# Moving half copies, sums, gates and one low half in a one-core attention and expert kernel

## What is computed

```
mask = q_bucket == k_bucket                 # 6 sign bits of q @ proj and of k @ proj
scores = where(mask, q @ k.T / 8, -1e9)
attn = exp(scores - max) / (sum + 1e-9);  x = attn @ v      # (1536, 512)
x = (sigmoid(x @ w_gate) * (x @ w_val)) @ w_out             # hidden width 1536
h = x @ w_in
g = where(h >= 1, h, where(h <= -1, 0, (h + 1)**2 / 4))     # hidden width 2048
out = g @ w_out2
```

## Time and profile before

| | |
|---|---|
| median of 3 runs | 792.86 us (792.75 to 793.1) |
| the profiled execution, its span | 792.82 us, 790.7 us |
| PE busy | 775.2 us, 98% |
| VectorE, ScalarE, GpSimd busy | 551.3 (70%), 461.5 (58%), 538.5 (68%) |
| chain that ended last | PE 79%, VectorE 6%, ScalarE 6%, issue 4%, GpSimd 4% |
| PE clock in 40 slices | 9 tenths or more in each |

### The profile page before, as it was taken

The page is one execution under the profiler, slowest core; times in us unless marked ns, Lnnn a source line. Parts: engine busy times, 40 slices in busy tenths (PEclk is TensorE's granted clock), DMA queues, the critical chain, the costliest instruction groups (busy, mean ns, idle before and its releaser), DMA issues.

```text
span 790.7 us, 12182 instructions
## 1 busy us (share of the span) xinstructions
PE 775.2 (98%) x4403; PEld 717.3 (91%) x4403; DVE 551.3 (70%) x862; ACT 461.5 (58%) x731; POOL 538.5 (68%) x533
## 2 busy tenths in 40 slices
PE   7999999999999999999999999999999999999998
PEld 6899999998989999999899999988899988899996
DVE  5888888888888666555765655577677776766554
ACT  4888988988997443344453334356455465634443
POOL 4567667778889988877596977747756755465420
PEclk9999999999999999999999999999999999999999
DMA  6895586385100222022021211121121011201002
GB/s 146 181 197 131 136 168 141 79 163 131 55 1 1 80 81 81 29 78 80 27 81 54 80 54 63 44 80 54 32 77 54 29 51 40 95 27 54 1 1 80
DMA packets 61930, 60.08 MB, mean 76 GB/s; under 512 B 28384, under 2 KB 51632, under 8 KB 61872
## 3 DMA queue, kind: packets, MB, share of 16 engines
q1 hardware_dynamic: 61712, 59.32, 28.5%
q10 hardware_dynamic: 160, 0.00, 0.0%
HBM read 37.75 MB, written 3.15 MB: 52 GB/s over the span
## 4 chain that ended last, share of the span: by engine, by line
PE 79%; DVE 6%; ACT 6%; issue 4%; POOL 4%; DMA 0%; SPq 0%; DVEq 0%; POOLq 0%; ACTq 0%
PE ps L748 12%; PE ps L749 11%; PE ps L750 11%; PE ps L777 8%; PE ps L789 5%; PE ps L790 5%; PE ps L788 5%; PE ps L778 4%; PE ps L714 4%; ACT ph L906 2%; PE ps L731 2%; PE ps L732 2%; PE ps L702 2%; DVE probs L1207 2%; PE ps L705 2%
## 5 line engine op out<-in xcount | busy, mean ns | idle before, releaser
L748 PE MATMUL ps<-xop,wset 128*128 128x384 f32 x560 | 191.0, 341 | 4.1 <-DVE u L1282 2.1
L749 PE MATMUL ps<-xop,wset 128*128 128x384 f32 x560 | 189.3, 338 | 0.0
L750 PE MATMUL ps<-xop,wset 128*128 128x384 f32 x560 | 188.8, 337 | 0.0
L1282 DVE TENSOR_TENSOR u<-ps,u 128x384 f32<-128x384 f32 x144 | 79.6, 553 | 109.0 <-PE ps L750 108.3
L516 POOL TENSOR_TENSOR wset<-stage,wset 128x512 fp32r<-128x512 f32 x39 | 56.5, 1448 | 112.7 <-ACT wset L953 112.7
L748 PEld LDWEIGHTS ps<-xop,wset 128*128 128x128 f32 x560 | 105.2, 188 | 18.0 <-issue 3.8
L1218 DVE TENSOR_TENSOR pl<-ps,ph 128x768 fp32r<-128x768 f32 x96 | 91.5, 954 | 26.5 <-ACT ph L906 25.4
L749 PEld LDWEIGHTS ps<-xop,wset 128*128 128x128 f32 x560 | 105.4, 188 | 3.5
L491 POOL TENSOR_SCALAR probs<-probs,small 128x768 f32<-128x768 f32 x96 | 88.4, 927 | 24.9 <-DVE small L1212 22.1
L750 PEld LDWEIGHTS ps<-xop,wset 128*128 128x128 f32 x560 | 105.2, 188 | 0.0
L522 POOL TENSOR_TENSOR wset<-wsum,wset 128x1024 fp32r<-128x1024 f32 x39 | 95.3, 2443 | 0.0
(11 more groups left out here) (134 smaller groups left out, 1710.4 us busy)
## 6 DMA issues: line engine op xcount, KB each, us to landing
stage<-in_moe_w_in_dram SPq DMA_DIRECT2D x16, 512.0 KB, 3.6
stage<-in_moe_w_out_dram SPq DMA_DIRECT2D x14, 512.0 KB, 3.6
stage<-in_moe_w_gate_dram SPq DMA_DIRECT2D x12, 512.0 KB, 4.3
stage<-in_moe_w_val_dram SPq DMA_DIRECT2D x12, 512.0 KB, 3.5
ops<-qh SPq DMA_DIRECT2D x15, 384.0 KB, 5.3
ops<-kh SPq DMA_DIRECT2D x28, 192.0 KB, 5.1
qn<-in_q_dram SPq DMA_DIRECT2D x16, 192.0 KB, 4.5
kn<-in_k_dram SPq DMA_DIRECT2D x16, 192.0 KB, 5.0
```

Of the source, the lines that this page charges most:

```text
L748: pe.matmul(dst, high[:, c, :], high_x(r)[:, c, :], start=(c == 0), stop=False)
L749: pe.matmul(dst, high[:, c, :], low_x(r)[:, c, :], start=False, stop=False)
L750: last = pe.matmul(dst, low[:, c, :], high_x(r)[:, c, :], start=False, stop=(c == 1))
L1282: dve.tensor_tensor(dst, bank(n, r), other, ALU.add).then_inc(e_dve, 1)
```

## The change

Seven edits. In attention ScalarE's `copy_half` for u = 5, 8, 11 moves from ahead of the step's cast and exponential to behind them; at u = 2 it stays ahead. In pair 5 GpSimd's three pieces of the first sums come at u = 1, 4, 7 instead of 4, 7, 10. GpSimd's `low_wo` of set 25 (f = 4) comes in set 26. In sets 24 and 32 ScalarE takes relu and square together ahead of the next set's first product, which goes back into that set, and VectorE adds the hinge ahead of the next set's bank 1. Value sets next to a first set gate their second half in two parts of 384 columns, the first of them ahead of `empty(n, 5)`. The sums ahead of the second and third first set (12 and 24) move from sets 3, 4, 5 behind a first set to 4, 6, 8.

```diff
-                if i == NP - 3 and u in (4, 7, 10):
-                    first_sum(0 if u == 4 else 2, (u - 7) // 3)
+                if i == NP - 3 and u in (1, 4, 7):
+                    first_sum(0 if u == 4 else 2, u // 7)
...
-                if WO2 + 1 < n <= WO2 + T2 + 1 and n % 2:
+                if WO2 + 1 < n <= WO2 + T2 + 1 and (n % 2 and n != N1 + 1 or n == N1 + 2):
                     f = (n - WO2 - 2) // 2
                     low_wo(T1 // 2 + f, f, (narrow2(2 * f), narrow2(2 * f + 1)))
...
             def hinge_set(n):
-                if n - 1 not in FIRSTS:
-                    first_product(n)
+                first_product(n)
                 if n in FIRSTS:
                     round_w(n + 1)
                     empty_y(g - 1)
-                    hinge_relu(t)
-                    first_product(n + 1)
-                    hinge_square(t)
+                    hinge_part(t)
                     return
...
-                if g % HT == 2 and g >= 11:
+                if u == 2 and g >= 11:
                     copy_half((g - 11) // HT)
...
                 exponential(g)
                 if g % HT == 2 and g >= 11:
+                    if u != 2:
+                        copy_half((g - 11) // HT)
                     copy_other((g - 11) // HT)
...
+            def gate_half(n):
+                two = hidden(pair_of(n), 1)
+                dve.wait_ge(sig_done, 2 * pair_of(n) + 1)
+                dve.wait_ge(*emptied(n, 4))
+                dve.tensor_tensor(two[:, G:S], two[:, G:S], tmp[:, G:S], ALU.mult)
+            def gate_other(n):
+                two = hidden(pair_of(n), 1)
+                dve.wait_ge(*emptied(n, 5))
+                dve.tensor_tensor(two[:, 0:G], two[:, 0:G], tmp[:, 0:G], ALU.mult).then_inc(gated, 1)
...
-                if g < 3 and n - FIRSTS[g] in (3, 4, 5):
-                    sum_x(g + 1, n - FIRSTS[g] - 3)
+                at = (4, 6, 8) if g < 2 else (3, 4, 5) if g == 2 else ()
+                if n - FIRSTS[g] in at:
+                    sum_x(g + 1, at.index(n - FIRSTS[g]))
...
                 empty(n, 4)
-                sum_ahead(n)
-                empty(n, 5)
                 if n - 1 in FIRSTS or n + 1 in FIRSTS:
-                    gate_second(n)
+                    gate_half(n)
+                    empty(n, 5)
+                    gate_other(n)
                     empty(n, 6)
                 else:
+                    empty(n, 5)
                     empty(n, 6)
                     gate_second(n)
...
                 empty(n, 6)
+                add_hinge(t)
                 if n in FIRSTS:
                     empty(n + 1, 1)
-                add_hinge(t)
                 clamp(t + 1)
```

More of the change, by code:

```diff
@@ L992, in sigmoids, with hinge_part @@
                     act.activation(hidden(pp, second), hidden(pp, second), ACT.Sigmoid).then_inc(sig_done, 1)
-            def hinge_relu(t):
+            def hinge_part(t):
                 act.wait_ge(clamped, t - TILES1 + 1)
                 act.activation(tile(t), tile(t), ACT.Relu, bias=minus_one).then_inc(hinge_parts, 1)
-            def hinge_square(t):
                 act.activation(tmp[:, :], tmp[:, :], ACT.Square, bias=half, scale=0.5).then_inc(hinge_parts, 1)
-            def hinge_part(t):
-                hinge_relu(t)
-                hinge_square(t)
             def empty_y(g):
```

## The result

The changed kernel takes 803.15 us (median of four runs, 802.77 to 804.83) against 792.81 (792.38 to 793.1) for the kernel before on the same chip: a ratio of 1.0137, interval 1.0122 to 1.0152. That is 1.2 us above the forecast of 802.0 and inside the range. The profiled execution took 803.02, with a span of 801.2 where the one before had 790.7. First the page: span, busy time by engine, and the chain of work that ended last.

What follows compares the result with a forecast made beforehand. TensorE, busy 98% of the span at full clock, was taken as the bound. Terms +2.8 - 0.95 + 2.3 - 0.7 - 0.9 + 6.6 = +9.15 on 792.86 gave 802.0 us, range 796 to 805.5.

Steps and rivals of the forecast that it cites:

- copies: Attention: ScalarE's moved half copies make the key turn late in six pairs, 0.46 us each; +2.8 us.
- first sums: Attention, pair 5: the GpSimd piece at u = 10 moves to u = 1, where the queue has room; -0.95 us.
- gate halves, sets 1 and 13: Each half gate waits for a whole GpSimd instruction, delaying PE's products; +1.4 and +0.9, together +2.3 us.
- sums ahead: VectorE's sums leave sets 3 and 5 for gate sets, where a down unit covers them; -0.7 us.
- hinge order, 24/25: Hinge addition ahead of the next set's bank shortens the chain at sets 24/25 by about 0.55 us.
- hinge order, 32/33: Hinge addition ahead of the next set's bank shortens the chain at sets 32/33 by about 0.35 us.
- low half moved: Set 26: GpSimd's later low half delays a weight load and ScalarE's cast, so PE waits twice; +6.6 us.
- first wait: Set 26: PE's third product waits for ScalarE's late copy of bank 0; 4.7 us.
- second wait: Set 26: PE then waits for a tile needing VectorE's addition, clamp, bank and subtraction; 1.9 us taken.
- B: Rival, attention: the copy's move fills PE's waits, giving 4.6 instead of taking 2.8; 794.6 us total, chance 0.10.
- C: Rival, SyncE's wait ahead of the sixth load: the moved low half holds nobody; 794.3 us total, chance 0.06.
- A: Rival, gate sets: halves are free, VectorE and GpSimd sharing in proportion; 799.4 us total, chance 0.12.

Runs made afterwards that it cites:

- e3: Kernel before with only the half copies of u = 5, 8, 11 moved behind the exponential; 796.49 us against 792.61, ratio 1.0040.
- e10: Kernel before plus earlier first sums, sums ahead, hinge order, and set 25's low half in GpSimd's gap ahead of low_a(26); 788.18 us against 792.4.
- e4: Kernel before with only the second gate of sets 1, 11, 13, 23 in halves; 794.9 us, ratio 1.0030.
- e5: Kernel before with only the hinge order of sets 24 and 32 changed; 792.99 us, ratio 1.0004.
- e1: Kernel before with only the low half of set 25 moved to set 26; 802.0 us against 792.61, ratio 1.0113.
- e7: Changed kernel plus 25 PE matmuls by zeros ahead of the waiting third product of set 26; 801.4 us, ratio 1.0110 to the kernel before.
- e9: Kernel before with only the half copy of u = 11 moved behind the exponential; 794.06 us against 792.4, ratio 1.0018.
- e6: Changed kernel with set 25's low half in GpSimd's gap ahead of low_a(26); 794.77 us, ratio 1.0029 to the kernel before.
- e2: Changed kernel with the low half back in set 25; 795.12 us, ratio 1.0036 to the kernel before.
- e12: Kernel before with gate halves, and GpSimd's 1024-wide subtraction of sets 2 and 14 in four of 256 columns; 794.28 us against 793.08, ratio 1.0018.
- e8: Kernel before with only the half copy of u = 5 moved behind the exponential; 795.11 us against 792.16, ratio 1.0030.
- e11: Kernel before with the half copies of u = 8 and 11 moved behind the exponential; 793.84 us against 792.4, ratio 1.0016.

## Why the prediction was right, step by step

| term | forecast | in the changed kernel | alone |
|---|---|---|---|
| copies | +2.8 | } +2.5 | +2.8 (e3) |
| first sums | -0.95 | } | -0.95 (e10) |
| gate halves, sets 1 and 13 | +2.3 | +2.1, some of it given back | +1.5 net (e4) |
| sums ahead | -0.7 | -1.2 | -1.3 (e10) |
| hinge order, 24/25 | -0.55 | -1.5 | -0.05 (e5), -1.1 (e10) |
| hinge order, 32/33 | -0.35 | -0.6 | -0.6 (e5) |
| low half moved | +6.6 | +8.8 | +9.1 (e1) |
| the end | 0 | +1.0 | +1.1 in all kernels with halves |

The third column comes to 11.1. The growth of the whole span is 10.5; of the 0.6 between, 0.4 is what the gate halves give back.

**The low half** had the right mechanism, stage by stage, and was 2.2 short. The first wait was sized well: I had 562.2 for the landing and a PE wait of 4.7, and by e7 the first wait is worth 4.55. The second wait, forecast at 1.9, is 2.5 there. Part of it is one row: the hinge addition behind the square lasted 1.51 us.

```profile
566.26 1.51 DVE L1323 TENSOR_TENSOR hid<-hid,tmp 128x768 f32<-128x768 f32 x1 [10.97 <-ACT tmp L998]
```

The missing rest, 1.7, is the clock, which has no term in my sum at all. The trace of before couldn't price it: its clock is 1.00 throughout, and PE has no idle of that length in it. The error was to cost a PE idle of nearly 5 us at its own length. My upper bound of 8.5 was too low for the same reason.

**Attention.** Each of the two terms is right alone to a tenth, and their sum was wrong: together +2.5 where they were to give +1.85. The first sums give 0.95 alone and only 0.35 beside the copies. The wait at the end of pair 5 is one for GpSimd. With the copies alone (e3) it is still there, and hides what the copies cost in this pair. In the changed kernel it has gone, and PE waits at the same turn for VectorE's subtraction instead:

```profile
187.68 0.85 PE L714 MATMUL ps<-ident,probs 128*128 128x128 f32 x6 [0.82 <-POOL probs L491]
```
```profile
187.89 0.85 PE L715 MATMUL ps<-ident,probs 128*128 128x128 f32 x6 [0.32 <-DVE pl L1212]
```

I added two terms that share a place. And the reason behind +2.8, the copy of u = 11 ahead of the next key turn, is the minor one: e9 gives it 0.14 a pair and some 0.5 once. I had written that the next query turn doesn't come earlier, and so let nothing pay for the late cast; in e9 it comes 0.4 earlier. The major one is u = 5. I had named the 0.91 us of idle time that hid this copy, and then not priced its leaving, because I counted four copies in the cycle from cast to cast in either order. The size came out right by luck of the sum. The pair's 29.6 us lies just above the 29.4 to 29.5 that I asked for. The turns in the pair of the earlier trace rows, with VectorE's subtraction of the turned queries ahead of them:

```profile
98.81 0.95 DVE L1179 SCALAR_TENSOR_TENSOR ql<-ps,qh 128x768 fp32r<-128x768 f32 x1
99.04 0.85 PE L715 MATMUL ps<-ident,probs 128*128 128x128 f32 x6 [0.29 <-DVE pl L1212]
99.91 0.30 PE L666 MATMUL ps<-ident,kn 128*128 128x128 f32 x1
```

The key turn starts at 99.91, 1.42 after the 98.49 of before, where the marks at the pair's start stand 0.95 apart: it is 0.5 late within its pair, where I had 0.3 to 0.4. The wait that makes it late, 0.29 us, stands ahead of the turn of probabilities before it.

**Gate halves.** PE's waits are where I put them, bank 5 first, then bank 6, then set 14's:

```profile
264.71 2.39 POOL L522 TENSOR_TENSOR wset<-wsum,wset 128x1024 fp32r<-128x1024 f32 x1
...
265.86 1.66 DVE L1302 TENSOR_TENSOR hid<-hid,tmp 128x384 f32<-128x384 f32 x1
...
268.02 1.05 DVE L1307 TENSOR_TENSOR hid<-hid,tmp 128x384 f32<-128x384 f32 x1
268.13 0.41 PE L749 MATMUL ps<-xop,wset 128*128 128x384 f32 x1 [1.01 <-DVE tmp L1276]
...
269.69 0.41 PE L749 MATMUL ps<-xop,wset 128*128 128x384 f32 x1 [0.25 <-DVE u L1276]
...
411.02 0.41 PE L749 MATMUL ps<-xop,wset 128*128 128x384 f32 x1 [0.66 <-DVE tmp L1276]
```

Forecast +1.4 and +0.9, measured +1.2 and +0.94. I hadn't seen that later waits give part of it back, some 0.1 and 0.3 here, 0.3 and 0.3 in e4.

**Sums ahead.** Sets 3 and 5 gave 0.9. A further 0.35 came in set 17, where I had written that PE doesn't idle. The trace of before shows no idle mark there, but its row has the sign that I overlooked, a product of 0.41 us where one that waited for nothing takes 0.34:

```profile
455.15 0.41 PE L748 MATMUL ps<-xop,wset 128*128 128x384 f32 x1
```

**Hinge order.** The direction held and the size was too small. At 24/25 the gain is mostly the clamp's, freed from the low half (0.9 by e1 against 0.05 for the order by itself), and with both it is 1.5 in the changed kernel, and 1.1 in e6 and e10, where the low half stands in GpSimd's gap. I had taken one term of 0.55 for the two.

**The end.** I had nothing for it, and it is +1.0. VectorE's last copy of an output starts at 796.92 of 801.2, so 4.3 us ahead of the end; in e10 at 782.87 of 786.1, 3.2 ahead:

```profile
796.92 0.69 DVE L1474 COPY x<-ps 128x512 f32<-128x512 f32 x1 [0.71 <-PE ps L791]
```
```profile
782.87 0.69 DVE L1464 COPY x<-ps 128x512 f32<-128x512 f32 x1 [0.71 <-PE ps L792]
```

All six kernels with gate halves (the changed one, e2, e4, e6, e7, e12) have 4.3 to 4.4, all eight without (before, e1, e3, e5, e8 to e11) the 3.2. In those six the queue that loads instructions moves a packet 1.8 us ahead of the end; in the other eight its last packet comes 100 us earlier. The DMA queues of the changed kernel from 796 to 802 us (packets, MB, share):

```profile
q14 instruction: 1, 0.01, 0.3%
```

The association is shown. That VectorE's eight additional instructions (four multiplications, four of its sequencer) push its code over the edge of one more block to load is an argument; no run took that block away and kept the halves.

The errors partly cancel: against the forecast's +9.15 the low half's +2.2, the end's +1.0 and attention's +0.65 are partly met by the hinge order (-1.2), the sums ahead (-0.5) and the gate halves (-0.6 net). So that the total came within 1.2 us of the forecast, where single terms miss by up to 2.2, is partly luck. Rivals B and C are ruled out by e3 and e1, A by e4 and e12.

## What to carry to other kernels

Before moving a cheap instruction to a quieter place, ask what its end releases: here 2.5 us of GpSimd's work, moved some 14 us later, held a buffer, the buffer a load, the load a cast, and the cast three instructions for which TensorE waited. The same instruction at another quiet place, ahead of the release, made the kernel faster. A TensorE idle of over 4 us cost more than its length here, one of 2.25 us in e7 was followed by no slower clock; so hide a long one, or add the slower clock behind it; and two terms of a sum that end at the same wait can't both be counted.

## What the runs showed of the hardware that I had not expected

- An idle of TensorE of 4.36 us was followed by 7.4 us at a granted clock of 0.57 and 0.51, worth 1.7 us; 25 matmuls by zeros in the wait kept the clock at 1.00.
- VectorE's clamp of 768 columns, with one input in SBUF, took 1.55 us beside GpSimd's low half and 0.56 without: not only instructions with two SBUF inputs are held up. The Trainium skill ("SBUF — State Buffer", "Who interferes with whom") names this kind of instruction among those that can take the shared port pair, and these rows agree.
- GpSimd's subtraction of 1024 columns takes 2.39 us as one instruction and 3.50 as four beside VectorE's gates, and VectorE's half gate beside it falls from 1.67 to 0.70.
- Eight more VectorE instructions came with 1.1 us at the end of the kernel, and with a packet of instruction loading 1.8 us ahead of the end; why is open.
